# Splitting the merge matmuls into two head groups, and the loads that come with it, in a packed-attention and feed-forward kernel

## The chip, the cores and the metric

The kernel runs on one NeuronCore of one Trainium2 chip; the other cores are idle. The metric is the device time of one execution in microseconds (us), taken as the median of several runs. Engines are named as in the profile: PE is TensorE (matrix multiply, PEld its weight loads), DVE is VectorE, ACT is ScalarE, POOL is GpSimd, SP is SyncE, which here only issues DMAs.

## The reference

```python
B, H, S, D = 8, 8, 576, 64            # batch, heads, sequence, head size; 32 packing queries
def sm_attn(qq, kk, vv):
    s = qq @ kk.T / sqrt(D)
    a = exp(s - max(s)); a = a / (sum(a) + 1e-9)
    return a @ vv
packed = sm_attn(p, k, v)             # (B, H, 32, 64)
x = sm_attn(q, packed, packed)        # (B, H, 576, 64) -> 4608 tokens x 512
h = x @ w_in                          # 4608 x 1024
e = exp(h - max(h)); sm = e / (sum(e) + 1e-9)
solu = h * sm
ln = (solu - mean(solu)) / sqrt(var(solu) + 1e-6) * g_ln
y = ln @ w_out                        # 4608 x 512
h2 = max(y @ w1, y @ w2, y @ w3)      # 4608 x 768
out = h2 @ w_out2                     # 4608 x 512
```

All inputs are float32. q, k, v are each 9.4 MB, 1152 KB for one batch.

## The kernel before

The program has three stages. The **attention stage** (to about 200 us) works batch by batch over the 8 batches. The **first feed-forward stage** takes 9 blocks of 512 tokens through `x @ w_in`, the softmax-like unit, the layer norm and `w_out`. The **second** forms `w1`, `w2`, `w3` with a Strassen scheme and ends with `w_out2`. The change touches the attention stage alone.

There the 8 heads of a batch stand as QUADS = 2 groups `g` of QH = 4 heads `h`. One group's scores fill 128 partitions: 4 heads x 32 packing queries. What a batch does, in the order in which its data is needed:

- **Loads (SP).** `load_k` brings k in two halves (`x`), `load_v` v and `load_q` q in one DMA each, into `k_raw`, `v_raw`, `q_raw`, one buffer each. Group 0 stands in partitions 0 to 63, group 1 in 64 to 127 (`half(g)`), and a partition holds 9 tokens of each of 4 heads, in runs of 2304 bytes. Before the change group g holds the heads 2h + g, so that one DMA over 128 partitions walks both groups. `p_raw` holds the packing queries, loaded twice, and `w_in` (2048 KB) is loaded once, behind q of batch 1.
- **Turns (PE).** `turn_k`, `turn_q`, `turn_p`, `turn_packed` transpose 128x128 pieces into two PSUM banks that are used in turn (0, 1); ACT or DVE copies each out (`copy_k`, `copy_q`, `copy_packedT`).
- **First attention.** `scores1(b, g)`, `max1` (DVE), `exp1` (ACT), `turn_a1`, and `pack(b)`, which multiplies by v; `take_packed` scales. The result, transposed, is `packedT`, a tile [128, 8 heads, 2, 32]: even heads of a pair have their 64 features in rows 0 to 63 and slot 1, odd heads in rows 64 to 127 and slot 0, and the rest is zero (a memset at the start).
- **Second attention.** `scores2(b, g)`, softmax over each head's 32 columns (DVE, POOL, ACT), `turn_out`.
- **Merge.** The packed values are multiplied by their head's rows of `w_in` before the attention weights are applied: `merge(b)` gives M = packed @ w_in, 4 heads x 32 rows by 1024 columns per group. Group 0 lands in the PSUM banks 4, 5 and group 1 in 6, 7 (`wide_banks`). ACT copies them out (`copy_m`), for batches 0 and 1 also DVE (`lo_m`), later ones go to DRAM (`store_merged`, POOL). `scores1(b + 2, g)` takes the same banks and waits for `m_copied[g]` (and `m_low` for b < 2).

`step(b)` sets by hand in which order PE works. It overlaps three batches: first half of batch b + 2 (`first`), the middle of b + 1 (`second`), and the rest of b (`third`). ACT, DVE and POOL have their own `step` in their own order. Every dependence is a semaphore, and each engine works strictly through its list; SP waits for a buffer to come free before it issues the next load, in the order k, p, v, q.

[...] Several matmuls that use different rows or columns of the array run at the same time: a tile of 64 rows by 32 columns takes an eighth of it.

Of the kernel before, what the change touches and what calls it, by code (L numbers as in the profile page):

```python
# [20 lines left out]
P = 128  # L21
B, H, S, D = 8, 8, 576, 64
NPACK = 32
PAIRS = H // 2
QUADS = H // 4
# [19 lines left out]
QH = H // QUADS  # L45
J = S // HALF
# [24 lines left out]
def packed_attention_ffn(nc, q, k, v, p, w_in, w_out, g_ln, w1, w2, w3, w_out2, out):  # L71
# [76 lines left out]
    pT = place("pT", [P, QUADS, P])  # L148
# [66 lines left out]
    wide_banks = (4, 6)  # L215
# [56 lines left out]
        wait(eng, sem, value)  # L272


    w_in_v = w_in.rearrange("(h p) n -> p h n", p=P)
    w_out_v = w_out.rearrange("(k p) n -> p k n", p=P)
    w_out2_v = w_out2.rearrange("(k p) n -> p k n", p=P)
    thirds = [w.rearrange("(k p) (m i n) -> p k m i n", p=P, m=2, n=P) for w in (w1, w2, w3)]
# [10 lines left out]
        return sum(16 if c < W2_END else 32 for c in range(n % 2, n + 1, 2))  # L289

    def rows(t):
        return t.rearrange("b (h g) (p j) d -> b (g p) h (j d)", g=QUADS, j=J)

    k_v, v_v, q_v = rows(k), rows(v), rows(q)
    p_v = p.rearrange("b (g q) n d -> b (q n) g d", g=QUADS)
# [1 line left out]
    def half(g):  # L297
        return slice(g * HALF, (g + 1) * HALF)

    def token_of(m):  # L300

        return J - 1 if m == 0 else 2 * ((m - 1) % STEPS) + (m - 1) // STEPS

    def main_cols(t, part, h, g):

# [99 lines left out]
    with block:  # L405

        @block.sync
        def _(sp):
            def load_k(b):

                if b > 0:
                    sp.wait_ge(kT_filled, (QH + 1) * b)
                for x in range(2):
                    at = slice(2 * x, 2 * x + 2)
                    sp.dma_start(k_raw[:, at, :, :].rearrange("p h j d -> p h (j d)"), k_v[b][:, at, :])\
                        .then_inc(k_loaded[x], 16)

            def load_p(b):

# [5 lines left out]
            def load_v(b):  # L425

                if b > 0:
                    sp.wait_ge(u_filled, b)
                sp.dma_start(v_raw[:, :, :, :].rearrange("p h j d -> p h (j d)"), v_v[b]).then_inc(v_loaded, 16)

            def load_q(b):

                if b > 0:
                    sp.wait_ge(qT_filled, (QH + 1) * b)
                sp.dma_start(q_raw[:, :, :, :].rearrange("p h j d -> p h (j d)"), q_v[b]).then_inc(q_loaded, 16)

            def load_in(b):

# [269 lines left out]
        def _(pe):  # L708
# [43 lines left out]
            def turn_k(b, j):  # L752
                bank = take_bank("k", b, j)
                if j % 2 == 0:
                    pe.wait_ge(k_loaded[min(j // 2, 1)], 16 * b + 16)
                turn_rows(bank, k_raw, j).then_inc(kT_filled, 1)

            def turn_p(b):
# [19 lines left out]
            def scores1(b, g):  # L778

                pe.wait_ge(*turn_done("k", b, QH))  # L780
                pe.wait_ge(*turn_done("p", b))
                if b == 1 and g == 1:

                    pe.wait_ge(packed_first, 1)
                    pe.wait_ge(packed_second, 1)
                elif b > 1:

                    pe.wait_ge(m_copied[g], b - 1)
                    if b < 4:
                        pe.wait_ge(m_low, QUADS * (b - 2) + g + 1)  # L790

                def small(jj, h):
                    n = QUADS * h + g
                    return pT[jj * D:(jj + 1) * D, n // QH, n % QH * NPACK:(n % QH + 1) * NPACK]

                scores(g, scores1_bank(g), small, kT).then_inc(s1_filled, 1)

# [9 lines left out]
            def turn_q(b, j):  # L807
                bank = take_bank("q", b, j)
                if j == 0:
                    pe.wait_ge(q_loaded, 16 * b + 16)  # L810
                turn_rows(bank, q_raw, j).then_inc(qT_filled, 1)

            def pack(b):

                pe.wait_ge(v_loaded, 16 * b + 16)
                pe.wait_ge(a1T_first, 2 * b + 2)
                pe.wait_ge(a1T_second, b + 1)
                for m in range(J):
                    for h in range(QH):
                        rows = slice(h * NPACK, (h + 1) * NPACK)  # L820
                        for g in range(QUADS):
                            last = pe.matmul(ps[rows, u_banks[g], 0:D], a1T[half(g), m, rows],  # L822
                                             v_raw[half(g), h, token_of(m), :], start=m == 0, stop=m == J - 1)
                last.then_inc(u_filled, 1)
# [19 lines left out]

                scores(g, scores_cols(mid_banks[0]), small, qT).then_inc(s2_filled, 1)

            def merge(b):
                pe.wait_ge(*turn_done("packed", b))
                if b == 0:
                    pe.wait_ge(w_in_loaded, 16)  # L850
                if b == B - 1:

                    for g in range(QUADS):
                        pe.wait_ge(m_copied[g], B - 1)
                else:

                    pe.wait_ge(packed_first, b + 2)
                    pe.wait_ge(packed_second, b + 2)
                    if b == B - 2:

                        pe.wait_ge(h_used, 1)
                for n in range(2):
                    for h in range(QH):
                        for g in range(QUADS):
                            last = pe.matmul(ps[h * NPACK:(h + 1) * NPACK, wide_banks[g] + n, :],  # L865
                                             packedT[b % 2][half(g), QH * g + h, 1 - g, :],
                                             w_in_s[half(g), h, n * 512:(n + 1) * 512], start=True, stop=True)
                            if n == 1 and h == QH - 1:
                                last.then_inc(m_filled[g], 1)

            def tile_terms(n):

# [43 lines left out]
            def step(b, third=True, second=True, first=True):  # L916
# [20 lines left out]
                    up(0, 0)  # L937
                if second:
                    turn_q(b + 1, 0)
                if second:  # L940
                    turn_q(b + 1, 1)
                    turn_packed(b + 1)
                if third and first:
                    merge(b)
                if second:
                    turn_q(b + 1, 2)
                if first:
# [6 lines left out]
                if first:  # L954
                    scores1(b + 2, 1)
                if third and not first:
                    merge(b)

            pe.wait_ge(ident_ready, 1)

# [51 lines left out]
            def last_step():  # L1012
                b = B - 1
                scores2(b, 0)
                up(0, 1)
                scores2(b, 1)
                merge(b)
                turn_h(0, 0)
                up(0, 2)
                turn_h(0, 1)  # L1020
                up(0, 3)
                turn_h(0, 2)
                up(1, 0)
                turn_h(0, 3)
                up(1, 1)
# [129 lines left out]
        def _(act):  # L1155
# [53 lines left out]
            def copy_m(b, g):  # L1209
                act.wait_ge(m_filled[g], b + 1)  # L1210
                if 2 < b < B - 1:

                    act.wait_ge(m_stored, 16 * (b - 2))
                dst = m_s[b][:, 0, g, :] if b < 2 else merged_of(b)[:, g, :]
                bank = wide_banks[g]
                copy(dst.rearrange("r (n c) -> r n c", n=WIDE), ps[:, bank:bank + WIDE, :]).then_inc(m_copied[g], 1)
# [11 lines left out]
            def step(b, third=True, second=True, first=True):  # L1228
# [25 lines left out]
                    exp_h(0, 0)  # L1254
                if third and first:
                    copy_m(b, 0)
                    copy_m(b, 1)
                if third and b < 2:
                    hi_a(b)
# [6 lines left out]
                    exp1(b + 2, 0)  # L1266
                if third and not first:
                    copy_m(b, 0)
                    copy_m(b, 1)


            act.wait_ge(zeroed, 4)
# [617 lines left out]
```

## Time and profile before

| | |
|---|---|
| Median of 3 runs | 1070.61 us (1068.88 to 1072.28) |
| Profiled execution: time, span | 1070.61 us, 1068.8 us |
| Mean granted clock of PE | 0.977 of full speed |
| PE busy | 1014.4 us (95%), 6626 matmul records |
| DVE, ACT, POOL busy | 57%, 32%, 23% |
| DMA, mean over the span | 171 GB/s |

The first 200 us are unlike the rest. After them PE is busy 862 of 869 us at full clock. In them it is busy 152 of 200 us, its granted clock is 0.88, and the DMA engines move 221 GB/s.

```profile
PE   7878876999999999999999999999999999999998
DMA  7867851434644446123565535454355535542341
```

These two lines give the busy share of the span in 40 equal slices, in tenths (9 is 90% or more), for PE and for the mean of the 16 DMA engines. A slice is 26.7 us; the attention stage is the first seven.

### The profile page before, as it was taken

Reading aid. Unit: us, or ns where it says so; the run is one execution under the profiler, and the core shown is the slowest. Engines: PE = TensorE matmul, PEld = TensorE weight load, DVE = VectorE, ACT = ScalarE, POOL = GpSimd, SP = SyncE. Lnnn points to the kernel's source line nnn. Section 1 sums busy time; section 2 is a strip of 40 time slices with the busy share of each in tenths; the row PEclk is TensorE's granted clock in tenths of the full one; section 3 lists DMA queues with packets and bytes.
Section 4 is the critical chain, followed back from the end, with each engine's and each line's share of the span. In section 5 each row is a group of like instructions: output and inputs, shape, how many; then the busy total and the mean of one; then the engine's idle time right before and its main releaser. Section 6 shows DMA issues by size and latency. Waiting matters only on the chain.

```text
span 1068.8 us, 16036 instructions
## 1 busy us (share of the span) xinstructions
PE 1014.4 (95%) x6626; PEld 813.0 (76%) x6626; DVE 605.5 (57%) x980; ACT 344.5 (32%) x551; POOL 250.8 (23%) x222
## 2 busy tenths in 40 slices
PE   7878876999999999999999999999999999999998
PEld 5544543778888888888888888888888888888887
DVE  2776756785666567756456553656365643663021
ACT  4645533243343243233322142223322241223111
POOL 0223553285794669360000000000000000000000
PEclk9889987999999999999999999999999999999999
DMA  7867851434644446123565535454355535542341
GB/s 247 308 227 274 286 173 63 163 99 160 216 163 159 145 153 239 79 119 109 204 259 206 177 110 213 172 184 176 137 184 205 206 109 187 206 142 86 117 159 40
DMA packets 46633, 183.24 MB, mean 171 GB/s; under 512 B 7520, under 2 KB 7520, under 8 KB 36960
## 3 DMA queue, kind: packets, MB, share of 16 engines
q1 hardware_dynamic: 40336, 147.20, 38.6%
q0 software_dynamic: 6224, 35.00, 9.0%
q8 instruction: 53, 0.87, 0.3%
q14 instruction: 20, 0.16, 0.0%
HBM read 134.62 MB, written 47.58 MB: 170 GB/s over the span
## 4 chain that ended last, share of the span: by engine, by line
PE 82%; DVE 8%; issue 4%; ACT 3%; DMA 2%; POOL 1%; ACTq 0%; POOLq 0%
PE ps L1082 27%; PE ps L716 25%; PE ps L1114 14%; PE ps L1105 5%; PE ps L730 3%; PE ps L983 2%; PE ps L865 1%; PE ps L822 1%; DVE h_lo L1473 1%; PE ps L774 1%; DVE spot L1770 1%; DMA q_raw<-in_q_dram 1%; PE ps L732 1%; DVE spot L1761 1%; DVE bn L1657 1%
## 5 line engine op out<-in xcount | busy, mean ns | idle before, releaser
L1082 PE MATMUL ps<-ys,slot 128*128 128x512 f32 x1512 | 345.7, 390 | 0.5
L1082 PEld LDWEIGHTS ps<-ys,slot 128*128 128x128 f32 x1512 | 283.2, 188 | 62.5 <-ACT spot L1157 3.9
L1761 DVE TENSOR_TENSOR spot<-ps,spot 128x512 f32<-128x512 f32 x108 | 74.3, 688 | 99.2 <-PE ps L1082 73.7
L1157 ACT ACTIVATE spot<-ps 128x512 f32<-128x512 f32 x90 | 52.8, 596 | 207.5 <-PE ps L1082 196.4
L716 PE MATMUL ps<-ln_hi,w_out_s_lo 128*128 128x512 f32 x280 | 109.0, 389 | 0.0
L716 PE MATMUL ps<-ln_lo,w_out_s_hi 128*128 128x512 f32 x280 | 108.9, 389 | 0.0
L716 PE MATMUL ps<-ln_hi,w_out_s_hi 128*128 128x512 f32 x280 | 108.9, 389 | 0.0
L1114 PE MATMUL ps<-w_out_s_lo,h_hi 128*128 128x512 f32 x216 | 84.0, 389 | 0.0
L1114 PE MATMUL ps<-w_out_s_hi,h_hi 128*128 128x512 f32 x216 | 84.0, 389 | 0.0
L1114 PE MATMUL ps<-w_out_s_hi,h_lo 128*128 128x512 f32 x216 | 84.0, 389 | 0.0
L1288 ACT ACTIVATE u<-ps,neg_max 128x1024 f32<-128x1024 f32 x36 | 40.2, 1116 | 125.4 <-DVE neg_max L1639 125.4
L1157 ACT ACTIVATE h_hi<-spot 128x512 fp32r<-128x512 f32 x54 | 33.8, 633 | 118.4 <-DVE spot L1770 87.3
L1647 DVE TENSOR_TENSOR u<-ps,u 128x1024 f32<-128x1024 f32 x36 | 44.1, 1224 | 45.6 <-ACT u L1288 45.4
L716 PE MATMUL ps<-m_even,a_even 128*128 128x512 f32 x240 | 62.2, 412 | 5.3 <-ACT merged_last L1157 5.3
L1637 DVE TENSOR_REDUCE row_max<-ps 128x1 f32<-128x1024 f32 x36 | 43.6, 1212 | 39.7 <-PE ps L716 39.7
L716 PEld LDWEIGHTS ps<-ln_lo,w_out_s_hi 128*128 128x128 f32 x280 | 52.5, 188 | 11.0
L716 PEld LDWEIGHTS ps<-ln_hi,w_out_s_hi 128*128 128x128 f32 x280 | 52.6, 188 | 10.9
L716 PEld LDWEIGHTS ps<-ln_hi,w_out_s_lo 128*128 128x128 f32 x280 | 52.6, 188 | 10.9
L1770 DVE TENSOR_TENSOR spot<-ps,spot 128x512 f32<-128x512 f32 x24 | 16.6, 692 | 76.1 <-PE ps L1082 76.1
L716 PEld LDWEIGHTS ps<-m_even,a_even 128*128 128x128 f32 x240 | 47.2, 199 | 16.1 <-issue 5.9
L716 PE MATMUL ps<-m_odd,a_odd 128*128 128x512 f32 x240 | 57.6, 391 | 1.5 <-DVE ln_lo L1473 1.5
L1473 DVE TENSOR_TENSOR ln_lo<-ps,ln_hi 128x1024 fp32r<-128x1024 f32 x36 | 41.7, 1214 | 26.5 <-ACT ln_hi L1157 26.5
(152 smaller groups left out, 1476.0 us busy)
## 6 DMA issues: line engine op xcount, KB each, us to landing
slot<-w_operands SPq DMA_DIRECT2D x36, 1792.0 KB, 7.2
w_operands<-stage POOLq DMA_DIRECT2D x18, 1024.0 KB, 4.9
k_raw<-in_k_dram SPq DMA_DIRECT2D x16, 576.0 KB, 5.1
v_raw<-in_v_dram SPq DMA_DIRECT2D x8, 1152.0 KB, 7.7
q_raw<-in_q_dram SPq DMA_DIRECT2D x8, 1152.0 KB, 8.1
y_features<-yst SPq DMA_DIRECT2D x9, 1024.0 KB, 4.5
y_raw<-y_features SPq DMA_DIRECT2D x9, 1024.0 KB, 5.3
out_dram<-spot SPq DMA_DIRECT2D x36, 256.0 KB, 2.1
```

The source lines that it names most:

```text
L716: last = pe.matmul(dst, w[a], x[z], start=start and c == 0 and e == 0, stop=stop and c == n - 1 and e == len(PASSES) - 1)
L730: last = pe.transpose(bank[:, c * P:(c + 1) * P], full[:, x, 2 * c:2 * c + 2, :], ident[:, :])
L1082: last = pe.matmul(ps[:, group_bank(g, k), :], w[:, a - 1, i, kk, :], ys[:, b, j, kk, :], start=n < 4 and kk == 0 and e == 0, stop=kk == K ...
L1105: last = pe.matmul(ps[:, group_bank(g, k), :], w[:, a, i, kk, :], ys[:, b, j, kk, :], start=h == 0 and kk == 0 and e == 0, stop=h == 1 and ...
L1114: last = pe.matmul(ps[:, out_bank(n), :], h2[a][:, c, j * P:(j + 1) * P], w_out2_s[z][:, c, :], start=(c == 0 and e == 0), stop=(c == K2 - ...
L1157: return act.activation(dst, src, ACT.Copy)
L1288: act.activation(u[:, i, :].rearrange("r (n c) -> r n c", n=WIDE), ps[:, bank:bank + WIDE, :], ACT.Exp, bias=neg_max[:, i:i + 1], accum_ou ...
L1473: return dve.tensor_tensor(dst, src, hi.bitcast(F32), ALU.subtract)
L1637: dve.tensor_reduce(row_max[:, c], ps[:, bank:bank + WIDE, :], AX.XY, ALU.max).then_inc(h_max, 1)
L1647: dve.tensor_tensor(u[:, i, :].rearrange("r (n c) -> r n c", n=WIDE), ps[:, bank:bank + WIDE, :], u[:, i, :].rearrange("r (n c) -> r n c", ...
L1761: dve.tensor_tensor(dst[:, :], a, b, op).then_inc(ready, 1)
L1770: dve.tensor_tensor(best[m][c][:, :], src, best[m][c][:, :], ALU.max).then_inc(ready, 1)
```

## The change

Three edits go together.

1. The heads are grouped otherwise: group g holds the heads 4g to 4g + 3 (`(g h)` for `(h g)`). Then a load can't walk both groups in one pattern, and each DMA of k, v and q becomes two, one for each group, each over 64 partitions. The count that PE waits for doubles (32 for 16). `scores1` picks its stationary operand by the new order, and `w_in` is read as before under another name.
2. `merge(b)` becomes `merge(b, g)`. It used to issue, for both groups, 16 matmuls of 64 rows by 32 columns (one head each). Now each group has 4 matmuls of 128 rows by 64 columns: a pair of heads in one operand, whose four 64x32 corners are two packed heads and two blocks of zeros. Each still streams 512 columns.
3. The two halves are placed apart. In `step`, PE runs `merge(b, 0)` between `turn_q(b + 1, 0)` and `turn_q(b + 1, 1)`, and `merge(b, 1)` where `merge(b)` was. In step 6 (`first` false) `merge(6, 1)` stands behind `turn_packed` and only `merge(6, 0)` stays at the step's end. ACT's `copy_m` follows in step 6.

```diff
     def rows(t):
-        return t.rearrange("b (h g) (p j) d -> b (g p) h (j d)", g=QUADS, j=J)
+        return t.rearrange("b (g h) (p j) d -> b g p h (j d)", g=QUADS, j=J)
+
+    def pair_of(t, pair):
+        return t[:, 2 * pair:2 * pair + 2, :, :].rearrange("c h t n -> c (h t n)")[:, NPACK:3 * NPACK]
...
                 for x in range(2):
-                    at = slice(2 * x, 2 * x + 2)
-                    sp.dma_start(k_raw[:, at, :, :].rearrange("p h j d -> p h (j d)"), k_v[b][:, at, :])\
-                        .then_inc(k_loaded[x], 16)
+                    for g in range(QUADS):
+                        sp.dma_start(k_raw[half(g), 2 * x:2 * x + 2, :, :].rearrange("p h j d -> p h (j d)"),
+                                     k_v[b, g][:, 2 * x:2 * x + 2, :]).then_inc(k_loaded[x], 16)
...
-                sp.dma_start(q_raw[:, :, :, :].rearrange("p h j d -> p h (j d)"), q_v[b]).then_inc(q_loaded, 16)
+                for g in range(QUADS):
+                    sp.dma_start(q_raw[half(g), :, :, :].rearrange("p h j d -> p h (j d)"), q_v[b, g])\
+                        .then_inc(q_loaded, 16)
...
-            def merge(b):
+            def merge(b, g):
+                bank = wide_banks[g]
                 pe.wait_ge(*turn_done("packed", b))
                 if b == 0:
                     pe.wait_ge(w_in_loaded, 16)
                 if b == B - 1:
-                    for g in range(QUADS):
-                        pe.wait_ge(m_copied[g], B - 1)
-                else:
+                    pe.wait_ge(m_copied[g], B - 1)
+                elif g == 1:
                     pe.wait_ge(packed_first, b + 2)
                     pe.wait_ge(packed_second, b + 2)
-                    if b == B - 2:
-                        pe.wait_ge(h_used, 1)
+                elif b == B - 2:
+                    pe.wait_ge(h_used, 1)
                 for n in range(2):
-                    for h in range(QH):
-                        for g in range(QUADS):
-                            last = pe.matmul(ps[h * NPACK:(h + 1) * NPACK, wide_banks[g] + n, :],
-                                             packedT[b % 2][half(g), QH * g + h, 1 - g, :],
-                                             w_in_s[half(g), h, n * 512:(n + 1) * 512], start=True, stop=True)
-                            if n == 1 and h == QH - 1:
-                                last.then_inc(m_filled[g], 1)
+                    for l in range(2):
+                        last = pe.matmul(ps[l * 2 * NPACK:(l + 1) * 2 * NPACK, bank + n, :], pair_of(packedT[b % 2], 2 * g + l),
+                                         w_in_s[:, 2 * g + l, n * 512:(n + 1) * 512], start=True, stop=True)
+                last.then_inc(m_filled[g], 1)
```

`load_v` is edited as `load_q` is; the calls of `merge` and `copy_m` move as the order below shows.

PE in step 3, the middle of a batch, before: L730 is a turn, L832 `turn_packed`, L865 the merge, L769 and L774 the scores of the batch that comes.

```order
L730 MATMUL ps<-ident,q_raw 128x128 x8
L832 MATMUL ps<-ident,packed 128x128 x2
L865 MATMUL ps<-w_in_s,packedT_108 32x512 x16
L730 MATMUL ps<-ident,q_raw 128x128 x4
L769 MATMUL ps<-kT,pT 32x64 x4
```

The same place after, where the turn is L737, `turn_packed` L838, the merge L870 and the scores L776.

```order
L737 MATMUL ps<-ident,q_raw 128x128 x4
L870 MATMUL ps<-w_in_s,packedT_108 64x512 x4
L737 MATMUL ps<-ident,q_raw 128x128 x4
L838 MATMUL ps<-ident,packed 128x128 x2
L870 MATMUL ps<-w_in_s,packedT_108 64x512 x4
L737 MATMUL ps<-ident,q_raw 128x128 x4
L776 MATMUL ps<-kT,pT 32x64 x4
```

Half of the merge now stands ahead of the second turn of q and of the turn of the packed values.

SP from the loads of batch 2 to `w_in`, before.

```order
L415 DMA k_raw<-in_k_dram 128x2x576 [waits kT_filled]
L415 DMA k_raw<-in_k_dram 128x2x576
L423 DMA p_raw<-in_p_dram 128x2x64 [waits pT_filled]
L423 DMA p_raw<-in_p_dram 128x2x64
L429 DMA v_raw<-in_v_dram 128x4x576 [waits u_filled]
L435 DMA q_raw<-in_q_dram 128x4x576 [waits qT_filled]
L459 DMA w_in_s<-in_moe_w_in_dram 128x4x1024
```

And after.

```order
L418 DMA k_raw<-in_k_dram 64x2x576 [waits kT_filled]
L418 DMA k_raw<-in_k_dram 64x2x576 x3
L426 DMA p_raw<-in_p_dram 128x2x64 [waits pT_filled]
L426 DMA p_raw<-in_p_dram 128x2x64
L433 DMA v_raw<-in_v_dram 64x4x576 [waits u_filled]
L433 DMA v_raw<-in_v_dram 64x4x576
L441 DMA q_raw<-in_q_dram 64x4x576 [waits qT_filled]
L441 DMA q_raw<-in_q_dram 64x4x576
L466 DMA w_in_s<-in_moe_w_in_dram 128x4x1024
```

Four loads have become eight, with the same bytes, and none fills more than 64 partitions but those of p and `w_in`.

## Rows read from the trace of the kernel before

**Rows 1.** Stretches: length, busy PE, PEld, DVE, ACT, POOL; clock, DMA share, GB/s.

```profile
20.92:39.59 18.67, 14.81 (x450) 10.89 (x448) 11.93 (x26) 9.93 (x22) 4.07 (x4) 1.00 0.97 360
...
20.92:155.80 134.88, 105.92 (x2379) 65.44 (x2383) 95.50 (x179) 70.31 (x137) 49.00 (x40) 0.90 0.75 263
```

**Rows 2.** DMA queues and issues, stretch 20.9 to 155.8: packets, MB, share; KB, landing.

```profile
q1 hardware_dynamic: 15488, 28.58, 59.4%
q0 software_dynamic: 1152, 6.55, 14.7%
...
q_raw<-in_q_dram SPq DMA_DIRECT2D x7, 1152.0 KB, 8.6
k_raw<-in_k_dram SPq DMA_DIRECT2D x12, 576.0 KB, 5.9
...
w_in_s<-in_moe_w_in_dram SPq DMA_DIRECT2D x1, 2048.0 KB, 12.1
```

**Rows 3.** Line L435, all loads of q: issue to landing.

```profile
DMA to landing us min/median/max: 5.6/8.1/9.8
```

**Rows 4.** Line L415, all half loads of k: issue to landing.

```profile
DMA to landing us min/median/max: 3.7/5.1/9.6
```

**Rows 5.** SP's issues in order of time: start, us, what.

```profile
20.92 0.88 SPq L415 DMA_DIRECT2D k_raw<-in_k_dram  x2
...
27.39 0.51 SPq L459 DMA_DIRECT2D w_in_s<-in_moe_w_in_dram  x1
```

**Rows 6.** The chain that ended last, to 210 us: start, us, what.

```profile
0.73 3.98 DMA k_raw<-in_k_dram
...
10.86 3.81 DMA k_raw<-in_k_dram
...
39.59 2.58 PE ps L865 x31
...
88.73 1.92 PE ps L742 x16
...
102.47 0.63 DVE qT L1511
...
106.94 0.63 PE ps L732 x4
...
122.41 0.32 DVE packedT L1529
...
126.91 9.81 DMA q_raw<-in_q_dram
```

**Rows 7.** Matmuls of PE in order of time, stretches around three merges.

```profile
101.10 1.95 PE L865 MATMUL ps<-w_in_s,packedT 64*32 64x512 f32 x32
...
118.70 1.45 PE L730 MATMUL ps<-ident,q_raw 128*128 128x128 f32 x8
...
139.28 3.67 PE L865 MATMUL ps<-w_in_s,packedT 64*32 64x512 f32 x32
```

**Rows 8.** What PE waited for, to 200 us: total, times, longest.

```profile
PE ps L822 <- issue: 12.2, 5, 4.6
...
PE ps L716 <- ACT merged_last L1157: 5.3, 1, 5.3
...
PE ps L730 <- DMA q_raw<-in_q_dram: 2.5, 1, 2.5
PE ps L769 <- ACT merged L1157: 2.4, 4, 0.7
...
PE ps L769 <- DVE m_odd L1473: 2.0, 1, 2.0
PE ps L769 <- DVE m_even L1473: 1.4, 1, 1.4
```

**Rows 9.** Step 6's end in order of time: ACT's copies, POOL behind them.

```profile
173.78 1.94 ACT L1157 ACTIVATE merged<-ps 128x1024 f32<-128x1024 f32 x2 [3.06 <-PE ps L865]
...
176.27 0.55 POOL L655 DMA_DIRECT2D m_merged<-merged  x1 [6.92 <-ACT merged L1157]
```

More of the change, by code:

```diff
@@ L272, in wait_alone @@
         wait(eng, sem, value)
-    w_in_v = w_in.rearrange("(h p) n -> p h n", p=P)
+    w_in_v = w_in.rearrange("(k p) n -> p k n", p=P)
     w_out_v = w_out.rearrange("(k p) n -> p k n", p=P)
@@ L428, in load_v @@
                     sp.wait_ge(u_filled, b)
-                sp.dma_start(v_raw[:, :, :, :].rearrange("p h j d -> p h (j d)"), v_v[b]).then_inc(v_loaded, 16)
+                for g in range(QUADS):
+                    sp.dma_start(v_raw[half(g), :, :, :].rearrange("p h j d -> p h (j d)"), v_v[b, g])\
+                        .then_inc(v_loaded, 16)
             def load_q(b):
@@ L434, in load_q @@
                     sp.wait_ge(qT_filled, (QH + 1) * b)
-                sp.dma_start(q_raw[:, :, :, :].rearrange("p h j d -> p h (j d)"), q_v[b]).then_inc(q_loaded, 16)
+                for g in range(QUADS):
+                    sp.dma_start(q_raw[half(g), :, :, :].rearrange("p h j d -> p h (j d)"), q_v[b, g])\
+                        .then_inc(q_loaded, 16)
             def load_in(b):
@@ L754, in turn_k @@
                 if j % 2 == 0:
-                    pe.wait_ge(k_loaded[min(j // 2, 1)], 16 * b + 16)
+                    pe.wait_ge(k_loaded[min(j // 2, 1)], 32 * b + 32)
                 turn_rows(bank, k_raw, j).then_inc(kT_filled, 1)
@@ L792, in small @@
                 def small(jj, h):
-                    n = QUADS * h + g
-                    return pT[jj * D:(jj + 1) * D, n // QH, n % QH * NPACK:(n % QH + 1) * NPACK]
+                    return pT[jj * D:(jj + 1) * D, g, h * NPACK:(h + 1) * NPACK]
                 scores(g, scores1_bank(g), small, kT).then_inc(s1_filled, 1)
@@ L809, in turn_q @@
                 if j == 0:
-                    pe.wait_ge(q_loaded, 16 * b + 16)
+                    pe.wait_ge(q_loaded, 32 * b + 32)
                 turn_rows(bank, q_raw, j).then_inc(qT_filled, 1)
             def pack(b):
-                pe.wait_ge(v_loaded, 16 * b + 16)
+                pe.wait_ge(v_loaded, 32 * b + 32)
                 pe.wait_ge(a1T_first, 2 * b + 2)
@@ L939, in step @@
                     turn_q(b + 1, 0)
+                if third and first:
+                    merge(b, 0)
                 if second:
@@ L942, in step @@
                     turn_packed(b + 1)
-                if third and first:
-                    merge(b)
+                if third:
+                    merge(b, 1)
                 if second:
@@ L956, in step @@
                 if third and not first:
-                    merge(b)
+                    merge(b, 0)
             pe.wait_ge(ident_ready, 1)
@@ L1016, in last_step @@
                 scores2(b, 1)
-                merge(b)
+                merge(b, 0)
+                merge(b, 1)
                 turn_h(0, 0)
@@ L1256, in step @@
                     copy_m(b, 0)
+                if third:
                     copy_m(b, 1)
```

1 line of the change is left out of this document (removed).

## The prediction

> **What bounds the kernel now.** I read the two busy lines first. PE is full from the eighth slice on, and none of the edited lines runs there, so the change can only move the attention stage and shift the rest as it stands. Next I read the table by stretch. From 20.92 to 155.80, from the issue of k of batch 2 to about where the last q lands, PE is busy 105.9 of 134.9 us and its clock is 0.90, so PE is not the only limit. The DMA engines are busy 0.75 of that time, and in the first 18.7 us of it, until the first merge, 0.97 at 360 GB/s [rows 1]. That is a full queue. Third come the chain of waits and PE's own waits. The loads stand in both: the first k (3.98 us), the second k (3.81), and near the end q, on which the chain spends 9.81 us and PE waits 2.5 [rows 6, 8]. Between them the chain alternates between PE's turns and merges, ACT's copies and DVE's copies of the second softmax. "issue" inside the stream of `pack` (12.2 us in 5 places) is time in which PE had nothing visible to wait for [rows 8].
>
> **Part 1, the loads.** The bytes stay. A load of k, v or q now fills 64 partitions at a time and its two parts stand one behind the other in SP's queue, where before one DMA filled 128.
>
> What a load costs today: a half load of k (576 KB) lands after 3.7 us at best, a q (1152 KB) after 5.6 [rows 3, 4]. 576 KB more cost 1.9 us, so 1.8 us are fixed and the rest goes at about 300 KB/us. No row shows a transfer into 64 partitions. One end is that it runs at the rate of today, the other that the rate falls with the partitions it fills, so that each of these transfers takes twice as long. Below nothing isn't possible: no byte and no wait is taken off the queue.
>
> The upper end, step by step:
> - Start. The first two k loads are on the chain, each with 1.9 us of transfer: 2 x 1.9 = +3.8.
> - Stretch 20.92 to 155.80. SP's queue was busy 59.4% of 134.9 = 80.1 us for 28.58 MB [rows 2]. Of these, 7 q, 7 v and 12 half k are 20 x 1152 KB = 23.6 MB, or 66.1 us. Idle, over all queues, were 0.25 x 134.9 = 33.7 us [rows 1]. Twice 66.1 needs 66.1 more: 66.1 - 33.7 = +32.4, if nothing else can run beside them. POOL's stores took 14.7% = 19.8 us [rows 2]. They read full 128 partitions in a queue of their own. If they run beside a half-filling load, +12.6 is left.
>
> So between 0 and +36. The first merge shows where it bites first. It waits for `w_in`, issued at 27.39 and landed 12.1 us later, that is at 39.49, and the merge starts at 39.59 [rows 2, 5, 6]. From 20.92 the queue had no gap (0.97), and three full loads stand ahead of `w_in`: k, v and q, 3456 KB, 9.9 us at the 23.6 MB in 66.1 us. Doubled, `w_in` lands about 10 us later, and at this point the first half of the merge now stands ahead of two turns. After it `w_out_raw` and the stores keep the queue full, and q, which was already late once, is late in most batches: 3456 KB need 19.8 us of a step that takes 19.1 (the merges at 101.10 and 139.28 are two steps apart [rows 7]).
>
> I take twice the time with the stores running beside: 3.8 + 12.6 = +16.4, and 3.6 more for loads that start only when their single buffer is free, so that some idle time can't be used: +20. I choose the upper end for the rate because the queue's parts are in order and each part addresses one half of the tile only, so nothing in this kernel fills the other half meanwhile. It is a choice, and the other end stays as a rival.
>
> The Trainium skill has a rule that speaks for this end. "SBUF — State Buffer", section "Door 1: The DMA port swizzle", says that partitions 0 to 63 reach only 8 of the 16 ports, and gives 196 GB/s against 328 for a transfer of 1 MiB. Its section "Can I just issue two DMAs to hit both halves?" answers no. By its figures the factor is 1.67 for 2, and an estimate of the sum would be 0.67 x 66.1 - 33.7 = +10.6 in the stretch and +2.5 at the start, +13 in all. No run here shows it yet.
>
> **Part 2, the merge matmuls.** A merge is 32 records in 1.95 us at full clock, and 3.67 where the clock was low [rows 7]. Eight tiles run abreast, so that is 4 rounds of 0.49 us. The nearest row for tiles of 128 rows is L742: 8 matmuls (16 records) in quarters of the columns, four abreast, 1.92 us, that is 4 rounds of 0.48 [rows 6]. The new merge has 16 records, two abreast: 8 rounds x 0.48 = 3.8 us, +1.9 for each batch at full clock and +3.7 at half. Lower bound: no more than now, if rounds overlapped further. Upper: no overlap, 7.7 us, +5.7. I take +1.9.
>
> What it gives back. The first half is copied by ACT while the second runs, so the scores of the batch to come no longer wait for the copy: 2.4 us in four batches, 1.4 and 2.0 in batches 0 and 1 [rows 8]. Batch by batch: batch 0: 1.9 - 1.4 = +0.5. Batch 1, where the clock changes on the way: 3.0 - 2.0 = +1. Batch 2: 1.9 - 0.6 = +1.3. Batch 3: 0, since DVE first reaches the second q copy at 102.47, having waited for the softmax, and PE waits for DVE until 106.94 [rows 6]; the extra lies in front of these waits. Batch 4: PE's turns end at about 120.2 [rows 7]. With half a merge at a low clock ahead, DVE's copies start a microsecond late: +1. Batch 5 at the low clock: 3.7 - 0.5 = +3.2. Sum +7, of which I count +6, since some of it falls into PE's waits for DVE as in batch 3. If that cover were gone, batch 3 would cost 1.9 too. The merge of batch 7 stands ahead of PE's wait of 5.3 us for ACT and costs nothing [rows 8].
>
> If the loads are late, most of this disappears under their wait, because the DMAs don't wait for the merge: +2 in place of +6.
>
> **Part 3, the end of step 6.** ACT's two copies take 1.94 us from 173.78, and POOL waits 6.9 us for them [rows 9]. One of them now runs earlier: -1.
>
> **Nothing else.** The doubled counts add no wait. Four more issues in a step (0.88 for two k issues [rows 5], so 1.8 us of SP) lie in the queue's own shadow: SP waits for buffers most of the time.
>
> **Sum.** 20 + 2 - 1 = +21. The profiled execution took 1070.61 us, 1.8 above its span, and is the median itself, so 1070.6 + 21 = about 1092.
>
> **Rivals.**
> - A, the forecast: half-filling loads run at half rate. 1092, own range 1080 to 1104. For it: a queue at 0.97, and a q that is late already. Against: no transfer of this shape in the trace.
> - B, the loads run as now. Then 6 - 1 = +5: 1075.6, own range 1071 to 1080. For it: the bytes are equal, the runs stay 2304 bytes, and nothing in the trace ties the rate of a transfer to the partitions it fills.
> - C, faster. Place: the first scores behind the merge (L769). The waits there, 2.4 + 1.4 + 2.0 = 5.8 us, and 1 us in step 6 go, and the new merge costs nothing because it falls into time in which PE waits for DVE or `w_in`. 1070.6 - 6.8 = 1063.8. It decides if loads keep their rate and the extra on the path is under 5.8. Against it: the sum above finds 4 to 7 us of extra net of these waits.
> - D, half rate and nothing runs beside: 3.8 + 32.4 + 2 - 1 = +37, 1108.
>
> Were the instruction stream's stalls ("issue", 12.2 us) to shift because PE has fewer instructions, each case moves by up to 4 us either way. That is in the ranges.
>
> **Numbers.** A 0.55, B 0.28, C 0.08, D 0.09. The range 1072 to 1108 leaves out C, a bit of B and half of D: about 0.18. A measurement of this kernel tells 0.3%, 3.2 us, from no change. Faster: C and a sliver of B, 0.09. Same (1067.4 to 1073.8): the lower part of B and some of C, 0.11. Slower: 0.80.
>
> **What would show it.** A: the best landing of a q near 9.4 us for its two parts (1.8 + 2 x 3.8) in place of 5.6, `w_in` landing near 50 us after the start, DMA share above 0.85 until the last q, waits of PE for q or v of several us in most batches, and the span behind the stage unchanged at 869 us. B: landings as now, a merge that starts near 39.6. Part 2: a group's half of the merge is 8 records in 1.9 us at full clock. Part 3: POOL's store of the merged values 1 us sooner behind the last half. Wrong would be a q that lands in 5.6 us (A falls), or a whole merge in 2 us (part 2 falls), or a stage that ends sooner than before.

## The result and the profile after

| | before | after |
|---|---|---|
| Median | 1070.68 us (4 runs, 1068.88 to 1072.28) | 1098.22 us (4 runs, 1094.13 to 1101.03) |
| Ratio, 95% interval | | 1.0254 (1.0219 to 1.0291) |
| Profiled execution, span | 1070.61, 1068.8 | 1094.80, 1093.2 |
| First k or q issue to last q landing, from batch 2 | 20.92 to 155.8 | 23.70 to 185.5 |

The change makes the kernel 27 us slower. The prediction was 1092 us in a range of 1072 to 1108. The profiled execution lies at the low end of the runs after; its own difference is 24 us.

The table by stretch of the changed kernel, with the columns of [rows 1]: the saturated part up to the first merge, the whole loaded stretch, and the last 868.8 us.

```profile
23.70:51.81 28.11, 19.10 (x443) 13.42 (x442) 10.73 (x23) 10.36 (x22) 3.46 (x3) 0.82 1.04 247
23.70:185.50 161.80, 124.84 (x2301) 72.97 (x2299) 97.41 (x181) 72.07 (x138) 49.80 (x40) 0.88 0.91 221
224.40:1093.20 868.80, 861.92 (x3923) 714.70 (x3922) 474.34 (x740) 249.62 (x375) 183.39 (x160) 1.00 0.44 159
```

The third row is the first thing to check. With the last 868.8 us of before, in which PE is busy 862.1 us, it agrees to 0.2 us, so all the loss lies ahead of it. The first row shows what it is: the DMA engines are as full as in [rows 1] (a share of 1.04; packets that overlap count twice), but move 247 GB/s in place of 360. The second shows that over the whole stretch they are busy 0.91 where they were 0.75, at 221 GB/s in place of 263.

DMA queues and issues of the changed kernel in that stretch, as [rows 2].

```profile
q1 hardware_dynamic: 16060, 28.90, 77.5%
q0 software_dynamic: 1152, 6.55, 12.0%
...
v_raw<-in_v_dram SPq DMA_DIRECT2D x14, 576.0 KB, 9.4
...
k_raw<-in_k_dram SPq DMA_DIRECT2D x24, 288.0 KB, 6.3
...
w_in_s<-in_moe_w_in_dram SPq DMA_DIRECT2D x1, 2048.0 KB, 16.4
```

SP's queue was busy 77.5% of 161.8 = 125.4 us for nearly the bytes that took 80.1 before (28.90 MB for 28.58): +45.3. POOL's stores took 19.4 us, as before (19.8). If all of the growth is put on the 66.1 us of k, v and q, their factor is (66.1 + 45.3) / 66.1 = 1.69. The trace's packets, counted one by one, give 1.62 for a byte: those of 2304 bytes, which only k, v and q have, took 65.1 us of the 16 engines for 23.59 MB before and 106.6 us for 23.92 MB after. The rest of the growth lies on the other loads of the queue. The median packet of 2304 bytes went from 93 to 175 ns. In slices of 0.25 us (from 20 to 180 us) in which such packets alone fill the engines, they move 386 GB/s before and 230 after, 1.68 times less.

The chain that ended last, changed kernel: start, us, what.

```profile
2.85 6.55 DMA k_raw<-in_k_dram
...
14.33 6.11 DMA k_raw<-in_k_dram
...
35.23 16.45 DMA w_in_s<-in_moe_w_in_dram
51.81 3.00 PE ps L870 x8
...
77.16 3.22 PE ps L870 x8
...
130.22 11.09 DMA q_raw<-in_q_dram
...
164.89 3.61 PE ps L870 x8
...
175.03 10.42 DMA q_raw<-in_q_dram
...
195.26 3.63 PE ps L870 x8
```

Read against [rows 6, 7], the loss can be followed down the stage. The first merge starts at 51.81, where it stood at 39.59: +12. The first half of the merge of step 5 starts at 164.89 against 139.28: +26. The last q is now on the chain as well, with 10.42 us. `w_in` stands on the chain with 16.45 us; before, PE's wait for it was hidden in "issue".

What PE waited for to 225 us, as [rows 8].

```profile
PE ps L828 <- issue: 17.4, 7, 4.9
PE ps L737 <- DMA k_raw<-in_k_dram: 10.4, 4, 6.0
PE ps L739 <- DVE qT L1517: 6.7, 7, 3.5
PE ps L737 <- DMA q_raw<-in_q_dram: 5.0, 2, 4.2
...
PE ps L870 <- DMA w_in_s<-in_moe_w_in_dram: 2.1, 1, 2.1
```

PE waits longer for k (5.4 before), q (2.5), and in the stream of `pack` (12.2). The row "L739 <- DVE qT" has grown as well, from 4.0 to 6.7 us. It hardly depends on the loads (pair_merge, with the loads of before, has 6.8) and matters below, together with the wait of the earlier turns for the same copy (`L737 <- DVE qT`, L730 before), which shrank from 2.0 to 0.3 us. The waits for the copy of the merged values that stood in [rows 8] have gone, save 1.2 and 1.4 us in batches 0 and 1.

### The profile page after: what moved, and what is told of

The parts are those of the page before. It is cut to its first block, busy times and chain, and to the rows that moved or that the text cites. A ratio compares the mean times of both kernels' runs of the same rounds, so it can differ in the third digit from the quotient of the medians.

```text
span 1093.2 us, 15814 instructions
## 1 busy us (share of the span) xinstructions
PE 1030.2 (94%) x6498; PEld 815.8 (75%) x6498; DVE 606.3 (55%) x980; ACT 345.6 (32%) x551; POOL 250.8 (23%) x222
## 4 chain that ended last, share of the span: by engine, by line
PE 78%; DVE 9%; DMA 5%; issue 4%; ACT 2%; POOL 1%; SPq 1%; ACTq 0%
PE ps L1088 27%; PE ps L723 24%; PE ps L1120 13%; PE ps L1111 4%; PE ps L737 2%; PE ps L988 2%; DMA q_raw<-in_q_dram 2%; PE ps L870 2%; DMA w_in_s<-in_moe_w_in_dram 2%; DVE a2T L1570 1%; DMA k_raw<-in_k_dram 1%; DVE h_lo L1479 1%; DVE spot L1776 1%; PE ps L828 1%; DVE spot L1767 1%
## 5 line engine op out<-in xcount | busy, mean ns | idle before, releaser
L723 PE MATMUL ps<-m_even,a_even 128*128 128x512 f32 x240 | 59.4, 399 | 2.0 <-ACT merged_last L1163 2.0
L723 PEld LDWEIGHTS ps<-m_even,a_even 128*128 128x128 f32 x240 | 45.0, 190 | 12.2 <-issue 2.7
```

The lines of the kernel that those rows point to most:

```text
L723: last = pe.matmul(dst, w[a], x[z], start=start and c == 0 and e == 0, stop=stop and c == n - 1 and e == len(PASSES) - 1)
```

## The experiments

### Which half of the change costs the time

**split_half**: the kernel before, each load cut at partition 64. `part` runs over two slices; the counts that PE waits for double. The same edit is made for v and q.

```diff
-                    sp.dma_start(k_raw[:, at, :, :].rearrange("p h j d -> p h (j d)"), k_v[b][:, at, :])\
-                        .then_inc(k_loaded[x], 16)
+                    for part in (slice(0, HALF), slice(HALF, P)):
+                        sp.dma_start(k_raw[part, at, :, :].rearrange("p h j d -> p h (j d)"), k_v[b][part, at, :])\
+                            .then_inc(k_loaded[x], 16)
```

> The kernel before, with each load of k, v and q issued as two DMAs, one for partitions 0 to 63 and one for 64 to 127. Heads, merges and order stay as before. If the loads that fill half the partitions are what the change costs: 1090 to 1096 us, the median packet of 2304 bytes' load nearly doubled, DMA share of the attention stage above 0.8, w_in landing after 15 us or more. If the merge matmuls and their place are the cost: 1070 to 1073, landings as before (q 5.6 to 9.8 us).

Measured: 1093.0 us, ratio 1.0213 (1.0196 to 1.0230). The loads alone cost 22.8 of the 27 us. The signs that the expectation names are there: the median packet of 2304 bytes takes 173 ns for 93, `w_in` lands after 18.2 us, and the DMA share is 0.98 (below).

**split_heads**: as many DMAs, cut between heads instead.

```diff
-                sp.dma_start(q_raw[:, :, :, :].rearrange("p h j d -> p h (j d)"), q_v[b]).then_inc(q_loaded, 16)
+                for x in range(2):
+                    at = slice(2 * x, 2 * x + 2)
+                    sp.dma_start(q_raw[:, at, :, :].rearrange("p h j d -> p h (j d)"), q_v[b][:, at, :])\
+                        .then_inc(q_loaded, 16)
```

> The kernel before, with as many DMAs as split_half (each load of k, v and q in two), but cut between heads, so that each still fills 128 partitions. If half-filling is the cost: 1070 to 1074 us, DMA share as before (0.75 in the loaded stretch). If the number of DMAs or SP's time to issue them is the cost: the same time as split_half, 1090 or more.

Measured: 1072.1 us, ratio 1.0010 (0.9995 to 1.0025). Twice as many DMAs cost nothing that can be told from zero.

**split_parity**: two DMAs of 64 partitions each, the even and the odd ones.

```diff
-                    for part in (slice(0, HALF), slice(HALF, P)):
+                    for part in (slice(0, P, 2), slice(1, P, 2)):
```

> The kernel before, with each load of k, v and q as two DMAs of 64 partitions, the even and the odd ones, so that each spans the whole tile. If the number of partitions that a DMA fills sets its rate, as the prediction put it: the same as split_half, 1090 to 1096 us. If it matters which partitions (the lower or upper half as one side of the memory): 1070 to 1075.

Measured: 1074.2 us, ratio 1.0033 (1.0015 to 1.0052). This is the experiment that tells the mechanism. The number of partitions is that of split_half; only which ones differ, and 19 of the 23 us are gone. So my reason in part 1, that the rate falls with the number of partitions, is wrong. The half does it. In the slices that these packets fill alone, split_parity moves 371 GB/s, split_heads 365 and split_half 232. The Trainium skill's page "SBUF — State Buffer", "Door 1: The DMA port swizzle", has the rule that fits: bit 6 of the partition number picks which of a cluster's two ports is used, so one half reaches 8 of 16. By the same formula every second partition reaches all 16. Its factor of 1.67 (328 against 196 GB/s) stands beside 1.62 and 1.68 here. split_parity also reads other rows of DRAM in each DMA than split_half does; changed_parity below, which keeps the DRAM side of the changed kernel and moves only the partitions that are written, takes this rival away.

The busy table of the three over the same window, 20 to 156 us: split_half, split_heads, split_parity in this order.

```profile
20.00:156.00 136.00, 99.84 (x2077) 63.92 (x2080) 83.78 (x157) 67.28 (x130) 39.75 (x33) 0.88 0.98 240
```

```profile
20.00:156.00 136.00, 108.43 (x2365) 66.64 (x2367) 95.86 (x179) 70.89 (x138) 46.31 (x38) 0.90 0.75 258
```

```profile
20.00:156.00 136.00, 106.35 (x2254) 66.55 (x2252) 94.68 (x178) 71.59 (x139) 44.88 (x37) 0.92 0.76 258
```

A DMA share of 0.98 at 240 GB/s against 0.75 and 0.76 at 258: more engine time and fewer bytes.

What is left of split_parity's 3.5 us may be SP's issues. The issues of q, split_half, split_heads and split_parity in this order (ns, min/median/max):

```profile
L439 SPq DMA_DIRECT2D q_raw<-in_q_dram x16: 595/599/637, 16.5 to 165.9; - x16
```

```profile
L439 SPq DMA_DIRECT2D q_raw<-in_q_dram x16: 367/420/712, 13.3 to 149.3; - x16
```

```profile
L439 SPq DMA_DIRECT2D q_raw<-in_q_dram x16: 601/613/657, 14.8 to 151.1; - x16
```

Both kinds with 64 partitions take 0.60 us to issue, the one with 128 takes 0.42 (0.37 in the kernel before). That this is the 3.5 us was not tested.

**two_queues**: the changed kernel, with group 1's loads moved from SP to ACT. ACT issues each where its own waits have shown the buffer to be free; shown for q. `load_1` issues one `act.dma_start` into `half(1)`.

```diff
                 copy_turned(qT[part, j * 512:(j + 1) * 512], turned("q", b, j)[part, :], "q", b, j)
+                if j == QH:
+                    load_1(b + 1, q_raw, q_v, q_loaded)
```

> The changed kernel, with the loads of group 1 issued by ACT instead of SP, each at the place in ACT's list where its buffer is known to be free, so that both halves of the tile can be filled at once from two queues. If a queue's fixed order is what keeps one half idle: most of the loss comes back, 1075 to 1085. If two transfers to the two halves don't overlap even from two queues (the Trainium skill, page 'SBUF — State Buffer', section 'Can I just issue two DMAs to hit both halves?', says that it gains only 6%): 1093 to 1100.

Measured: 1096.0 us, ratio 1.0235 (1.0211 to 1.0260). The interval overlaps that of the change, so two queues bring nothing that the times can tell. The trace says a little more. From 20 to 180 us k, v or q packets of both queues were in flight together for 63 us, so both halves were being filled at once. Where nothing else moved and the engines were full, they made 263 GB/s together and 234 when one queue ran alone, 12% more, and far from the 386 of whole loads. The Trainium skill's 6%, which the expectation names, is of that order. ACT also has four more issues in a step, which this run doesn't separate from the rest.

### The merges

**pair_merge**: the changed kernel with the loads and groups of before.

```diff
-        return t.rearrange("b (g h) (p j) d -> b g p h (j d)", g=QUADS, j=J)
+        return t.rearrange("b (h g) (p j) d -> b (g p) h (j d)", g=QUADS, j=J)
```

> The changed kernel with the loads and head groups of the kernel before: pair-form merges in two halves, placed as in the change. The rows of w_in that a merge reads then belong to other heads, so the values differ; work, sizes and order are those of the change. By the prediction's rival B: 1075 us (1071 to 1080), each half of a merge 1.9 us. If the merge is free or gives more than it costs (rival C): 1064 to 1070. If it carries a large part of the 27 us: over 1085.

Measured: 1072.1 us, ratio 1.0009 (0.9996 to 1.0023). With split_half it makes 24 of the 27 us. The merge side costs about 1 us, less than rival B's +5.

**pair_together**: pair_merge with both halves where the merge stood before, so that the form alone differs.

```diff
-                if third and first:
-                    merge(b, 0)
                 if second:
                     turn_q(b + 1, 1)
                     turn_packed(b + 1)
-                if third:
-                    merge(b, 1)
+                if third and first:
+                    merge(b, 0)
+                    merge(b, 1)
```

> pair_merge with both halves of the merge at the old place (step 6 included), so that only the form of the matmuls differs from the kernel before; values as in pair_merge. By the prediction's sum the form alone costs 1.9 us a batch where nothing covers it, 1076 to 1082, and the placement gives back what pair_merge (1072) lacks to it. If the placement gives nothing: 1072.

Measured: 1068.0 us, ratio 0.9970 (0.9957 to 0.9984). My expectation missed: the form adds nothing to the time, and the placement gives nothing back but costs 4 us (1.0009 against 0.9970). PE's waits to 200 us, pair_merge and then pair_together:

```profile
PE ps L735 <- DVE qT L1514: 6.8, 7, 3.5
PE ps L867 <- DMA w_in_s<-in_moe_w_in_dram: 3.5, 1, 3.5
...
PE ps L772 <- DVE m_odd L1476: 1.4, 1, 1.4
PE ps L772 <- DVE m_even L1476: 1.4, 1, 1.4
...
PE ps L733 <- DVE qT L1514: 0.7, 1, 0.7
```

```profile
PE ps L735 <- DVE qT L1514: 4.3, 5, 3.0
...
PE ps L733 <- DVE qT L1514: 2.0, 1, 2.0
...
PE ps L772 <- DVE m_even L1476: 1.0, 1, 1.0
...
PE ps L772 <- DVE m_odd L1476: 0.2, 1, 0.2
```

The waits behind the merge, which I credited to the placement, are just as short with both halves together. What shortens them is that group 0 is finished before group 1 begins, so its copy runs beside group 1's matmuls. The old form finished both groups at once. Placed ahead of the turns, group 0's half delays the second turn of q and the turn of the packed values, and DVE's row of copies and `turn_out` behind them. PE meets this at its last turn of q: 6.8 us in 7 places against 4.3 in 5. But the wait for DVE at an earlier turn is shorter, 0.7 against 2.0, so together these rows explain 1.2 of the 4 us. The other place is step 0, where the first half now waits 3.5 us for `w_in` ahead of two turns: `pack` of batch 2 starts at 57.3 us in pair_merge and at 55.3 in pair_together. No run puts the halves apart in steps 1 to 5 alone, so how the 4 us divide between the two is open.

Nor do the runs show why the longer form costs nothing. At full clock a whole merge takes 3.65 us in pair_together and 1.95 before. Waits for DVE can cover it. But the clock differs too. The first 200 us, before and pair_together:

```profile
0.00:200.00 200.00, 152.28 (x2703) 98.47 (x2704) 130.13 (x240) 94.87 (x176) 67.34 (x62) 0.88 0.63 221
```

```profile
0.00:200.00 200.00, 158.56 (x2577) 97.87 (x2578) 130.41 (x240) 94.89 (x176) 67.36 (x62) 0.92 0.64 222
```

PE is busy 6.3 us longer, at a granted clock of 0.92 for 0.88. Work done at the full clock instead of half may pay for the extra rounds; no experiment separates this from the waits.

**w_in_late**: the changed kernel, with both halves behind the turns in step 0 alone.

```diff
-                if third and first:
+                if third and first and b > 0:
                     merge(b, 0)
                 if second:
                     turn_q(b + 1, 1)
                     turn_packed(b + 1)
+                if b == 0 and third:
+                    merge(b, 0)
```

> The changed kernel, but in step 0 alone both halves of the merge stand behind the turns, as before the change. split_half (+22) and pair_merge (+1) add up to 23 of the 27 us. If the rest comes from the first merge, which now waits for the late w_in ahead of two turns and of DVE's work behind them: 2 to 4 us less than the changed kernel, about 1095. If it is spread over all steps: no change from 1098.

Measured: 1093.0 us, ratio 1.0195 (1.0178 to 1.0213). The changed kernel's is 1.0254 (1.0219 to 1.0291) and the two intervals don't meet: by the middle values 6 us come back, where 2 to 4 were expected. By the times, the wait for `w_in` in front of two turns is where loads and placement make each other worse. That is more than the 3 us by which 22.8 + 1 falls short of 27. The traces don't show where the 6 us come back: the spans of the profiled executions are 1093.2 and 1091.3 us, and the last `pack` begins at 180.2 and 180.0. "issue" in `pack`'s stream takes 21.8 us in w_in_late's and 17.4 in the other, which may hide part of it.

### Repairs

**changed_parity**: the changed kernel with group g of k and q in the partitions of parity g.

```diff
-                    sp.dma_start(q_raw[half(g), :, :, :].rearrange("p h j d -> p h (j d)"), q_v[b, g])\
+                    sp.dma_start(q_raw[g:P:2, :, :, :].rearrange("p h j d -> p h (j d)"), q_v[b, g])\
...
-        return t[part, h * STEPS * P:(h + 1) * STEPS * P].rearrange("r (t g p) -> r g t p", t=STEPS, g=QUADS)[:, g]
+        return t[part, h * STEPS * P:(h + 1) * STEPS * P].rearrange("r (t p g) -> r g t p", t=STEPS, g=QUADS)[:, g]
```

> The changed kernel, with group g of k and q in the partitions of parity g instead of in one half; v stays in halves, since its matmuls need them. The scores then read every second column of the turned tiles. Two thirds of the bytes go at full rate: if the half is the cause, 27 - 2/3 x 22 = +12, about 1083 us, or less if v alone leaves the queue idle enough (1076). If not: 1098. If PE reads every second column more slowly: over 1085 with longer matmuls of the scores.

Measured: 1078.5 us, ratio 1.0056 (1.0040 to 1.0073): 20 us come back, more than two thirds of 22.8. Each DMA reads the same DRAM as in the changed kernel and only the partitions that it writes are others, so it is the SBUF side that costs. The queue has gaps again: from 20 to 156 us the DMA share is 0.83, where the changed kernel has 0.96. The longest matmuls of the scores, 256 columns, take 384 to 386 ns where every second column is read and 376 in the changed kernel, so this side costs PE little.

**changed_best**: changed_parity with both halves behind the turns in steps 0 to 5.

```diff
-                if third and first:
-                    merge(b, 0)
                 if second:
                     turn_q(b + 1, 1)
                     turn_packed(b + 1)
+                if third and first:
+                    merge(b, 0)
```

> changed_parity with both halves of the merge behind the turns in steps 0 to 5 (step 6 apart, as in the change). changed_parity took 1078.5 us. The placement cost 4 us with the loads of before and 5 in the changed kernel: 1073 to 1075. If v in halves is what is left: no less than 1073; if the placement costs nothing here: 1078.

Measured: 1073.0 us, ratio 1.0025 (1.0011 to 1.0038), as expected. What is left over the kernel before may lie in its waits (to 225 us): k is waited for longer (5.4 before), and v, still loaded in halves, and `w_in` are now waited for as well.

```profile
PE ps L737 <- DMA k_raw<-in_k_dram: 8.5, 4, 5.0
...
PE ps L870 <- DMA w_in_s<-in_moe_w_in_dram: 4.3, 1, 4.3
...
PE ps L828 <- DMA v_raw<-in_v_dram: 2.0, 1, 2.0
```

**step6**: the kernel before, with group 1 of step 6's merge behind `turn_packed` and ACT's copy with it.

```diff
+                if third and not first:
+                    merge(b, (1,))
                 if second:
                     turn_q(b + 1, 2)
...
                 if third and not first:
-                    merge(b)
+                    merge(b, (0,))
```

> The kernel before with one edit: in step 6 group 1 of the merge stands behind turn_packed and its copy goes with it. The prediction's part 3 alone: -1 us, 1069 to 1070. If the end of step 6 isn't on the path: no difference.

Measured: 1070.2 us, ratio 0.9999 (0.9984 to 1.0015): no difference by the times. The trace does show the microsecond. The two halves of step 6's merge, the copy and POOL's store in step6's trace:

```profile
161.95 1.92 PE L865 MATMUL ps<-w_in_s,packedT 64*32 64x512 f32 x16
...
169.88 3.64 PE L865 MATMUL ps<-w_in_s,packedT 64*32 64x512 f32 x16
...
173.58 1.02 ACT L1159 ACTIVATE merged<-ps 128x1024 f32<-128x1024 f32 x1 [3.01 <-PE ps L865]
174.91 0.55 POOL L655 DMA_DIRECT2D m_merged<-merged  x1 [5.70 <-ACT merged L1159]
```

From the copy's start to the store are 1.33 us, where [rows 9] have 2.49. A gain of 1.2 us is under what these intervals can tell. In the old form each half takes as long as the whole merge did (1.92 us for 16 records at full clock and 3.64 at the low one, beside 1.95 and 3.67 for 32 in [rows 7]), so this edit also gives PE one more such stretch and saves none in front of the copy.

**nat_pair**: the form and the loads of the kernel before together. The loads and the first attention stay on heads 2h + g; DVE's copy sorts the packed values by head; the second attention and the merges take heads 0 to 3 and 4 to 7, so `w_in` needs no other order.

```diff
-                scores(g, scores_cols(mid_banks[0]), small, qT).then_inc(s2_filled, 1)
+                scores(g, scores_cols(mid_banks[0]), small, qT,
+                       lambda h, g: divmod(QH * g + h, QUADS)).then_inc(s2_filled, 1)
...
-                    last = dve.tensor_copy(packedT[b % 2][part, :, 1 - jj, :], src[part, :, :])
+                    last = dve.tensor_copy(packedT[b % 2][part, :, 1 - jj, :].rearrange("c (m g) n -> c g m n", g=QUADS),
+                                           src[part, :, :].rearrange("c (g m) n -> c g m n", g=QUADS))
```

> The kernel before with its loads and its first attention unchanged, the packed values sorted by head when they are copied, the second attention and the merges done for heads 0 to 3 and 4 to 7, merges in the pair form, both halves at the old place. It is pair_together with the right rows. If pair_together's 0.3% is real: 1066 to 1069 us. If it was drift between runs: 1070 to 1072.

Measured: 1069.3 us, ratio 0.9990 (0.9974 to 1.0006). That is between my two cases. Its interval overlaps that of pair_together; together they say that the form is free or gains up to 0.3%, not that it gains 0.3%.

**nat_pair6**: nat_pair, with the halves apart in step 6, and ACT's copy of group 1 with its half.

```diff
+                if third and not first:
+                    merge(b, 1)
                 if second:
                     turn_q(b + 1, 2)
...
                 if third and not first:
                     merge(b, 0)
-                    merge(b, 1)
```

> nat_pair, with the two halves apart in step 6 alone, as the change has them. By part 3 of the prediction the store of the merged values and POOL's chain behind it start 1 us sooner, and there are 3 to 4 us of merge fewer in front of ACT's copy: 1 to 3 us under nat_pair. If POOL's w_out work sets that end anyway: no difference.

Measured: 1066.5 us, ratio 0.9968 (0.9954 to 0.9983). This version beats both kernels, by 0.3% and by 2.8%. The chain at step 6's end, nat_pair and then nat_pair6:

```profile
169.27 5.79 PE ps L868 x16
175.09 1.03 ACT merged L1161
```

```profile
167.03 3.64 PE ps L868 x8
170.69 1.03 ACT merged L1162
```

8 records stand ahead of ACT's copy in place of 16, 2.2 us fewer. The copy starts 4.4 us sooner, but the other 2.2 us stand already ahead of the edit: the last `pack` begins at 154.3 and 152.1. The medians are 2.8 us apart, within the 1 to 3 expected, though the two intervals against the kernel before still overlap. So in this kernel the placement seems to help in step 6, where group 1's half falls into PE's wait for DVE.

## Why the prediction was right, and where it was not

1. **The stage.** Right. The last 868.8 us are the same, and in the stage the load queue is what the change fills (0.91 for 0.75).
2. **Part 1, the size.** The time moved as forecast, 27 us for 21. The loads alone are 22.8 by split_half against my +20. But that is in part luck: three terms were off, and one was missing. The factor is 1.62 to 1.69 and not 2: +45.3 us of queue time for +66.1. The stores didn't hide behind the half-filling loads: in the slices of 0.25 us in which both moved (17 us in all) they made 325 GB/s. Halves alone made 233 in this stretch and stores alone 375, and by turns in the same shares they would make 314 (an estimate from these rates). So hardly anything of the 19.8 us I took off was saved. And of the 33.7 us of idle time 14.6 are still idle (0.09 x 161.8), where I had allowed 3.6, most likely since with one buffer each a load can't start before its turn. In sum: 45.3 - 0.4 - (33.7 - 14.6) = 26 of the 26.9 us by which the stretch grew, and it starts 2.8 later (mine: 3.8). My terms made 66.1 - 33.7 - 19.8 + 3.6 = 16 of this. PE needs only part of the 26, because the last q used to land at 155.8 and was taken at 160.4; this term I didn't have, and it brings 26 + 2.8 back to 22.8, near my 20.
3. **Part 1, the reason.** Wrong. I made the rate depend on how many partitions a transfer fills. split_parity fills as few and loses 3.5 us, not 23. The Trainium skill's page that I cited beside it, "SBUF — State Buffer", "Door 1: The DMA port swizzle", has the reason that fits, and its factor of 1.67 is nearer than my 2. The sum that I worked out from it, +13, is all the same further from 22.8 than my +20, since it lets all of the idle time be used.
4. **Part 1, the place.** Right: `w_in` landed at 51.6 (35.23 + 16.4; I said near 50) and the first merge followed. The best landing of a q, for which I named 9.4 us, can't be read, since its two DMAs overlap. Another sign missed: I named waits for q or v in most batches. PE waits for k instead, 10.4 us in 4 places, for q in 2 and for v never.
5. **Part 2, the matmuls.** Eight records of a half take 1.94 us at full clock, where 1.9 was said (below). But the step from there to the path fails. I charged the extra 1.9 us to the path in five of six batches (+6) and credited the placement with the waits that go. pair_together has the extra and is not slower, so something covers it. I had seen DVE's row behind the softmax do so in batch 3 and should have asked the same of the others; whether it is that or the higher granted clock (0.92 for 0.88) stays open. pair_merge shows the sign of the placement the other way round, +4. The two errors leave +1 where I had +6 alone, +2 under late loads.
6. **Interaction.** Not in the prediction: the early half in step 0, behind a late `w_in`, costs some 6 us by the times (w_in_late). I had named the place, but put the merges under the loads' cover only.
7. **Part 3.** In step6's trace, 1.2 us; in its times, not to be told.

The merge of step 3 in the changed kernel, in two halves around a turn. A half is 4 matmuls, and each stands in the trace as two records:

```profile
98.94 1.94 PE L870 MATMUL ps<-w_in_s,packedT 128*64 128x512 f32 x8
100.81 0.66 PE L737 MATMUL ps<-ident,q_raw 128*128 128x128 f32 x4
101.30 0.38 PE L838 MATMUL ps<-ident,packed 128*128 128x128 f32 x2
101.61 1.94 PE L870 MATMUL ps<-w_in_s,packedT 128*64 128x512 f32 x8
```

Of the rivals, B is refuted by split_half and D by the factor. C is refuted by split_half too, since the loads don't keep their rate; its other half, a merge that costs nothing, is what pair_together and nat_pair show, without the placement. Open is why "issue" in `pack`'s stream grew from 12.2 to 17.4 us. Over the runs it goes from 8.8 us (changed_parity) to 21.8 (w_in_late), and no experiment took it apart.

## What to carry to other kernels

When a layout is regrouped, look first at what the DMAs of it become. Here each of two transfers into the two halves of the partitions took 0.81 to 0.85 of the queue time that one into all of them took (1.62 / 2 and 1.69 / 2); if a split can't be avoided, cut between runs or by parity, not at partition 64. An engine's extra work is charged to the path only where the chain of waits passes through it in that very step: here 1.7 us more of merge a batch cost nothing, while running half of it earlier, ahead of what DVE and the next turns were waiting for, cost 4 us in all.

## What the runs showed of the hardware

- A load into partitions 0 to 63 or 64 to 127 takes 1.62 (packets alone) to 1.69 times the queue time of the same bytes into 128. Where the engines are full of such packets the rate is 230 GB/s for halves, 371 for every second partition and 365 to 386 for all 128.
- Issuing the two halves from two engines' queues lets them run together at 263 GB/s, 12% more than one queue at that time, and gains nothing that the times can tell (1096 us against 1098).
- SP takes 0.60 us to issue a load of q into 64 partitions, halves or parity, and 0.37 to 0.42 for one into 128.
- PE reads every second column of the turned tiles (changed_parity) in 384 to 386 ns for a record of 256 columns, where neighbouring columns take 376.
- At full clock 8 records of merge matmuls with 128 rows by 64 columns take 1.94 us (two abreast), 16 with 64 rows by 32 columns 1.92 (four abreast, step6), and 32 of the latter 1.95 (eight abreast).
